# First transfers of an attention and two-MLP kernel cut smaller, weight splits moved to other turns

## What is computed

```python
scores = np.where(mask, scale * q @ k.T, -1e9)          # mask: 0 <= i - j < 64
attn = exp(scores - max); attn = attn / (sum(attn) + 1e-9)
x = attn @ v                                             # as 1152 x 512
h = x @ w_in
x = (np.maximum(h, 0) + np.log1p(np.exp(-np.abs(h)))) @ w_out
p = domain_probs / (domain_probs.sum(-1) + 1e-9)
out = sum(p[:, e:e+1] * (np.maximum(x @ w1[e], 0) @ w2[e]) for e in range(4))
```

## Time and profile before

| | us |
|---|---|
| median of 3 runs (lowest, highest) | 632.37 (631.67, 632.61) |
| the profiled execution | 631.56 |
| its span, first to last instruction | 629.8 |
| TensorE busy | 621.8 (99%) |
| VectorE busy | 388.0 (62%) |
| ScalarE busy | 276.7 (44%) |
| GpSimd busy | 88.9 (14%) |

### The profile page before, as it was taken

How to read it: one execution, slowest core, us unless ns; L and a number is a source line. 1 busy time by engine, 2 the same in 40 slices (tenths; PEclk the granted TensorE clock), 3 DMA queues, 4 the chain that set the end, 5 groups by cost and what they waited for, 6 DMA issues and landing times.

```text
span 629.8 us, 10144 instructions
## 1 busy us (share of the span) xinstructions
PE 621.8 (99%) x3892; PEld 579.0 (92%) x3892; DVE 388.0 (62%) x840; ACT 276.7 (44%) x635; POOL 88.9 (14%) x92
## 2 busy tenths in 40 slices
PE   8999999999999999999999999999999999999998
PEld 7789999999999999998998988988988988988987
DVE  5896674577646588887277277276276376376342
ACT  6986765566445455552342332332332432432410
POOL 2653333323333332000000000000000000000000
PEclk9999999999999999999999999999999999999999
DMA  8814130123100010022102103003003003000012
GB/s 330 348 68 193 69 135 1 35 100 138 64 2 0 1 35 34 1 68 101 35 0 101 34 1 104 31 1 110 25 1 122 12 2 131 4 0 1 1 51 100
DMA packets 10704, 40.78 MB, mean 65 GB/s; under 512 B 1312, under 2 KB 1568, under 8 KB 9376
## 3 DMA queue, kind: packets, MB, share of 16 engines
q1 hardware_dynamic: 10656, 40.13, 17.7%
HBM read 37.77 MB, written 2.36 MB: 64 GB/s over the span
## 4 chain that ended last, share of the span: by engine, by line
PE 94%; ACT 1%; DVE 1%; DMA 1%; issue 1%; SPq 0%; POOL 0%; DVEq 0%; ACTq 0%
PE banks L1123 31%; PE banks L1099 28%; PE banks L1068 16%; PE banks L1048 15%; PE banks L1035 1%; DMA unit_in<-in_units 1%; PE banks L1009 1%; PE banks L1022 1%; ACT prob L498 1%; PE banks L1115 0%; DVE sp_l L734 0%; DVE prob L684 0%; ACT hid_hi L539 0%; ACT probT L507 0%; ACT sp_l L534 0%
## 5 line engine op out<-in xcount | busy, mean ns | idle before, releaser
L1123 PE MATMUL banks<-wb_hi,ehid_hi 128*128 128x512 f32 x284 | 110.5, 389 | 0.0
L1123 PE MATMUL banks<-wb_lo,ehid_hi 128*128 128x512 f32 x284 | 110.5, 389 | 0.0
L1123 PE MATMUL banks<-wb_hi,ehid_lo 128*128 128x512 f32 x284 | 110.5, 389 | 0.0
L431 POOL TENSOR_TENSOR sp_c<-sp_e,sp_c 128x384 f32<-128x384 f32 x48 | 63.6, 1324 | 135.3 <-DVE sp_c L720 135.3
L862 DVE SCALAR_TENSOR_TENSOR part<-banks,gate,part 128x512 f32<-128x512 f32 x62 | 46.6, 751 | 54.0 <-PE banks L1123 54.0
L1099 PE MATMUL banks<-T_lo,aop_hi 128*128 128x288 f32 x256 | 75.6, 295 | 0.0
L1099 PE MATMUL banks<-T_hi,aop_lo 128*128 128x288 f32 x256 | 75.6, 295 | 0.0
L1099 PE MATMUL banks<-T_hi,aop_hi 128*128 128x288 f32 x256 | 75.3, 294 | 0.0
L1068 PE MATMUL banks<-hid_hi,wb_hi 128*128 128x384 f32 x192 | 65.8, 342 | 0.8 <-DVE wb_lo L672 0.7
L1048 PE MATMUL banks<-xy_hi,wa_hi 128*128 128x384 f32 x192 | 66.3, 345 | 0.0
L1068 PE MATMUL banks<-hid_hi,wb_lo 128*128 128x384 f32 x192 | 64.3, 335 | 0.0
(11 more groups left out here) (106 smaller groups left out, 1247.5 us busy)
## 6 DMA issues: line engine op xcount, KB each, us to landing
unit_in<-in_units SPq DMA_DIRECT2D x8, 1024.0 KB, 6.3
raw_a<-in_w SPq DMA_DIRECT2D x16, 512.0 KB, 3.3
raw_b<-in_w SPq DMA_DIRECT2D x16, 512.0 KB, 3.3
raw_a<-in_w_in SPq DMA_DIRECT2D x8, 512.0 KB, 6.0
raw_b<-in_w_out SPq DMA_DIRECT2D x8, 512.0 KB, 4.2
part<-in_units SPq DMA_DIRECT2D x2, 1024.0 KB, 12.1
out_dram<-part SPq DMA_DIRECT2D x8, 256.0 KB, 2.0
unit_in<-in_units SPq DMA_DIRECT2D x2, 384.0 KB, 7.7
```

The source lines that it names most:

```text
L431: pool.tensor_tensor(sp_c[:, s, :], sp_e[:, s, :], sp_c[:, s, :], ALU.subtract).then_inc(lost_done, 1)
L1123: m = pe.matmul(TOKEN_BANKS[T], ehid[x][:, i, P * T:P * T + P], wb[a][:, f, :], start=(i == 0 and j == 0), stop=(i == 3 and j == 2))
```

## The change

1. In memory, a unit's keys (256 columns) now stand in front of its queries (384). Unit 0's inputs come in two pieces: keys and the first window's queries (192 KB), then the other queries (128 KB). Units 1, 2 and 3 each have a transfer of 320 KB. Groups 2 and 3 come in two pieces each, 640 KB and 384 KB, with the values later.
2. Unit 0's three windows go into three banks, and TensorE counts `first_scores` behind windows 0 and 1, so VectorE masks each window by itself.
3. The high copies of `wa` move from the turns 4, 5, 7, 8, 9 to 5, 6, 8, 9 and a last one behind turn 9, and GpSimd's epsilons and low halves move with them.
4. GpSimd waits in step 0 for unit 10's normalisation, and does block 4's second half in step 1. Block 5 is split by ScalarE in step 1 and by GpSimd in step 2, no longer by ScalarE and VectorE in step 3.
5. VectorE does `activation(0, 0)` in step 1, behind masked_scores(11).

```diff
-SPLIT_GROUPS = 2
+SPLIT_GROUPS = 4
+SINGLE = 4
+FIRST_QK = UNIT + WIN + P
...
+        def score_block(u, w):
+            bank = (score_bank(0), ps[1], ps[2])[w] if u == 0 else score_bank(u)
+            return bank[:, P * w:P * w + P]
...
-        FIRST_SPLIT = {4: 0, 5: 1, 7: 2, 8: 3, 9: 4}
+        FIRST_SPLIT = {5: 0, 6: 1, 8: 2, 9: 3}
-        LATE_SPLIT = {3: 5, 4: 6, 5: 7}
+        LATE_SPLIT = {4: 6, 5: 7}
...
-            sp.dma_start(slots[0][:, 0:UNIT_QK], units[0][:, 0:UNIT_QK]).then_inc(first_unit_landed, 16)
-            sp.dma_start(slots[0][:, UNIT_QK:2 * UNIT_QK], units[0][:, UNIT_QK:2 * UNIT_QK]).then_inc(scores_landed[0], 16)
-            first_queries_keys(1)
+            sp.dma_start(slots[0][:, 0:FIRST_QK], units[0][:, 0:FIRST_QK]).then_inc(first_window_landed, 16)
+            sp.dma_start(slots[0][:, FIRST_QK:UNIT_QK],
+                         units[0][:, FIRST_QK:UNIT_QK]).then_inc(unit_scores_landed[0], 16)
+            for u in range(1, SINGLE):
+                unit_queries_keys(u)
             first_values(0)
-            attention_inputs(2)
+            first_queries_keys(2)
             first_values(1)
-            attention_inputs(3)
+            first_queries_keys(3)
+            first_values(2)
             up_weights(0, up_in(0), (0,))
             attention_inputs(4)
+            first_values(3)
             up_weights(0, up_in(0), (1,))
...
-            for u in (2, 3, 4):
+            for u in (2, 3, 4, 5):
                 add_eps(u)
-            for i, unit in enumerate((4, 5, 6, 7)):
-                add_eps(unit + 1)
-                if unit in FIRST_SPLIT:
+            for i, unit in enumerate((5, 6, 7, 8)):
+                if unit + 1 in EPS_AHEAD:
+                    add_eps(unit + 1)
+                if i < 2:
                     pool.wait_ge(wa_hi, FIRST_SPLIT[unit] + 1)
                 else:
                     pool.wait_ge(norm_done, unit + 1)
                 up_low_half(i // 2, i % 2)
...
+            for i in range(4, 8):
+                pool.wait_ge(norm_done, SCORED)
+                if i % 2 == 0:
+                    pool.wait_ge(wa_hi, i // 2 + 1)
                 up_low_half(i // 2, i % 2)
             for k in range(STEPS):
                 lost(k // FT, k % FT)
                 if k == 0:
+                    pool.wait_ge(norm_done, SCORED + 1)
                     pool.wait_ge(wb_hi, 1)
                     down_low_half(0)
                     down_low_half(1)
-                    pool.wait_ge(wa_hi, len(FIRST_SPLIT))
-                    up_low_half(len(FIRST_SPLIT) - 1, 0)
-                    up_low_half(len(FIRST_SPLIT) - 1, 1)
+                    pool.wait_ge(wa_hi, 5)
+                    up_low_half(4, 0)
                 elif k < N_UNITS - SCORED:
                     normalise(k + SCORED)
+                if k == 1:
+                    up_low_half(4, 1)
+                elif k == 2:
+                    pool.wait_ge(wa_hi, 6)
+                    up_low_half(5, 0)
+                    up_low_half(5, 1)
...
+                if k == 1:
+                    act.wait_ge(wa_hi, 5)
+                    split_up(0, 5)
...
+                    if u == 0 and w < 2:
+                        dve.wait_ge(first_scores, w + 1)
+                    elif u == 0:
+                        dve.wait_ge(score_done, 1)
...
+            up_high(4)
...
+                if k == 1:
+                    activation(0, 0)
...
+                    if u == 0 and w == 1:
+                        pe.wait_ge(unit_scores_landed[0], 16)
+                    if u == 0 and w < 2:
+                        m.then_inc(first_scores, 1)
```

More of the change, by code:

```diff
@@ L189, in two_stage_mlp_after_window_attention @@
         qk_slots = [i[:, 0:2 * UNIT_QK].rearrange("p (t n) -> p t n", t=2) for i in slots]
-        q_slots = [i[:, :, 0:3 * P].rearrange("p t (w c) -> p t w c", w=3) for i in qk_slots]
-        k_slots = [i[:, :, 3 * P:UNIT_QK] for i in qk_slots]
+        q_slots = [i[:, :, UNIT + WIN:UNIT_QK].rearrange("p t (w c) -> p t w c", w=3) for i in qk_slots]
+        k_slots = [i[:, :, 0:UNIT + WIN] for i in qk_slots]
         v_slots = [i[:, Q_COLS + K_COLS:SLOT].rearrange("p (w c) -> p w c", w=3) for i in slots]
@@ L242, in two_stage_mlp_after_window_attention @@
         unit_landed = [sem(f"unit_landed{i}") for i in range(SLOTS + EARLY)]
-        scores_landed = [sem(f"scores_landed{g}") for g in range(SPLIT_GROUPS)]
-        first_unit_landed = sem("first_unit_landed")
+        scores_landed = {g: sem(f"scores_landed{g}") for g in (2, 3)}
+        first_window_landed = sem("first_window_landed")
+        unit_scores_landed = [sem(f"unit_scores_landed{u}") for u in range(SINGLE)]
         gate_in = sem("gate_in")
@@ L250, in two_stage_mlp_after_window_attention @@
         negmax_done = sem("negmax_done")
+        first_scores = sem("first_scores")
         first_maxima = sem("first_maxima")
@@ L319, in _, with unit_queries_keys @@
             QK = Q_COLS + K_COLS
+            def unit_queries_keys(u):
+                cols = slice(UNIT_QK * (u % 2), UNIT_QK * (u % 2) + UNIT_QK)
+                sp.dma_start(slots[u // 2][:, cols], units[u // 2][:, cols]).then_inc(unit_scores_landed[u], 16)
             def first_queries_keys(g):
@@ L458, in _ @@
                 up_low_half(i // 2, i % 2)
-            for i, unit in zip(range(len(FIRST_SPLIT) - 1, 2 * len(FIRST_SPLIT) - 2), (8, 9, 9, 9)):
-                pool.wait_ge(norm_done, unit + 1)
-                if i == 4:
-                    pool.wait_ge(wa_hi, 3)
-                elif i == 6:
-                    pool.wait_ge(wa_hi, 4)
+            for i in range(4, 8):
+                pool.wait_ge(norm_done, SCORED)
+                if i % 2 == 0:
+                    pool.wait_ge(wa_hi, i // 2 + 1)
                 up_low_half(i // 2, i % 2)
@@ L675, in masked_scores @@
             def masked_scores(u):
-                dve.wait_ge(score_done, u + 1)
+                if u > 0:
+                    dve.wait_ge(score_done, u + 1)
                 if u >= 3:
@@ L683, in masked_scores @@
                     m = 0 if first and w == 0 else 1
-                    e = dve.tensor_tensor_reduce(prob[:, u % 3, w, :], score_bank(u)[:, P * w:P * w + P],
+                    if u == 0 and w < 2:
+                        dve.wait_ge(first_scores, w + 1)
+                    elif u == 0:
+                        dve.wait_ge(score_done, 1)
+                    e = dve.tensor_tensor_reduce(prob[:, u % 3, w, :], score_block(u, w),
                                                  mask[:, m, :], -SCALE, BIG, ALU.add, ALU.min,
@@ L911, in _ @@
                         x_low(k + WEIGHED)
-                activation(n, f)
+                if k > 0:
+                    activation(n, f)
                 if n >= 1 and f == LAG - 1:
@@ L1000, in scores @@
                 if u == 0:
-                    pe.wait_ge(first_unit_landed, 16)
+                    pe.wait_ge(first_window_landed, 16)
+                elif u < SINGLE:
+                    pe.wait_ge(unit_scores_landed[u], 16)
                 elif u < 2 * SPLIT_GROUPS:
@@ L1008, in scores @@
                 for w in range(3):
-                    m = pe.matmul(score_bank(u)[:, P * w:P * w + P], q_slots[s][:, u % 2, w, :],
+                    if u == 0 and w == 1:
+                        pe.wait_ge(unit_scores_landed[0], 16)
+                    m = pe.matmul(score_block(u, w), q_slots[s][:, u % 2, w, :],
                                   k_slots[s][:, u % 2, WIN * w:WIN * w + P], start=True, stop=True)
+                    if u == 0 and w < 2:
+                        m.then_inc(first_scores, 1)
                 m.then_inc(score_done, 1)
@@ L1214 @@
                 v, 1 - h, 0)[3 * u:3 * u + 3, :, P * hp0:P * hp0 + 2 * P].transpose(1, 0, 2)
-        qk[:, :, :3 * P] = qh.reshape(P, 2, 3 * P)
-        qk[:, :, 3 * P:] = np.roll(k, WIN - UNIT * u, 2)[hp0:hp0 + 2, :, :UNIT + WIN].transpose(1, 0, 2)
+        qk[:, :, UNIT + WIN:] = qh.reshape(P, 2, 3 * P)
+        qk[:, :, :UNIT + WIN] = np.roll(k, WIN - UNIT * u, 2)[hp0:hp0 + 2, :, :UNIT + WIN].transpose(1, 0, 2)
         at[:, :Q_COLS + K_COLS] = qk.reshape(P, 2 * UNIT_QK)
```

## The result

The changed kernel took 632.61 us (median of 22 runs, 632.21 to 635.0); the kernel before, run beside it, 632.10 (22 runs, 631.42 to 632.99).

What follows compares the result with a forecast made beforehand. TensorE, busy 621.8 of 629.8 us, bounds the kernel; only gains ahead of its group at 45.65, waiting on VectorE, count. 0.60 - 0.15 = 0.45 us earlier gives 631.1 profiled, plus 0.81 for the median: 631.9; range 630.7 to 633.2.

Steps and rivals of the forecast that it cites:

- Unit 0: Start of kernel: VectorE's first mask starts behind the first window, 0.45 us sooner; lead at unit 0's maxima 0.43.
- Units 2 and 4: First transfers: smaller pieces land unit 2 near 6.3 and unit 4 at 10.1; lead 0.54, then 0.9 us.
- Units 4 to 7: Exponentials on ScalarE: unit 4 at 12.5, 1.75 us a unit, unit 7 at 17.75; lead 1.2 us.
- the second rival: Early lead under about 0.7 at unit 7, low halves come late; end 0.65 to 1.3 us later; chance 0.15.
- the wait on `wa_lo`: Sign: TensorE waits about 1 us on `wa_lo` ahead of `start_up(0, 0)` at 20.2.
- the late cast: Sign: third `raw_a` issued near 24.2, VectorE's cast at about 27.6, where 26.8 was before.
- unit 4's scores at 10.1: Sign: TensorE starts unit 4's scores near 10.1 us, a lead of 0.9.
- unit 7's exponentials at 17.7: Sign: ScalarE's exponentials of unit 7 come near 17.7 us, a lead of 1.2.
- Where the lead goes: GpSimd's low halves behind later units: scores(9) unchanged, third `raw_a` issued 0.9 us later; lead becomes a lag of 0.9.
- (a): Step 0: GpSimd waits for unit 10's normalisation, VectorE's epsilon and normalisation shorten; gain 0.84 us, lag left 0.05.
- (b): Step 1: `activation(0, 0)` behind mask 11 brings the mask earlier, but `split_up(0, 5)` delays unit 11's exponential; gain 0.
- (c): Block 5's low half moves from VectorE's step 3 to GpSimd's step 2: 0.60 us gained, 0.15 cost.

Runs made afterwards that it cites:

- e17: Kernel before with only unit 0's scores put in three banks and counted window by window; ratio to before 1.0001.
- e4: Changed kernel with both GpSimd low halves of a block together, the second ahead of the next unit's epsilon; 631.83 us, ratio to before 1.0002.
- e10: e4 with block 5 split in step 3 by ScalarE and VectorE as before the change; 631.92 us, ratio to before 0.9997.
- e2: Changed kernel's order on all engines (casts, low halves, late steps, block 5), but the kernel before's transfers; 633.08 us, ratio to before 1.0024.
- e7: Kernel before with block 1's second low half on GpSimd right behind its first, ahead of unit 8's epsilon; ratio to before 1.0.
- e1: Kernel before plus GpSimd's wait for unit 10's normalisation, `activation(0, 0)` behind mask 11, and block 5's low half off VectorE's step 3; ratio 1.0001.
- e6: e1 with block 5 split by ScalarE and VectorE in step 3 as in the kernel before; 631.26 us, ratio to before 0.999.
- e11: e3 plus GpSimd's wait for unit 10's normalisation, block 4's second half in step 1 and `activation(0, 0)` behind mask 11; 631.12 us, ratio 0.9987.
- e18: e6 plus unit 0's scores counted by windows, every transfer as in the kernel before; 631.12 us, ratio to before 0.9987.
- e9: Changed kernel with block 5 split in step 3 by ScalarE and VectorE as before the change; 632.74 us, ratio to before 1.0013.
- e12: e3 with group 1's queries and keys in one transfer of 640 KB; ratio to before 1.0006.
- e14: Kernel before with unit 0's queries and keys in two pieces, plus keys-first layout and scores by windows; ratio to before 1.0006.
- e15: e11 with unit 0's queries and keys in one whole transfer; 630.84 us, ratio to before 0.9987.
- e13: e3 with unit 0's queries and keys in one transfer of 320 KB; ratio to before 0.9989.
- e3: Kernel before with only the change's smaller transfers and unit 0 in two pieces with scores by windows; ratio to before 0.9998.
- e5: e3 with SyncE held back from issuing more until unit 2's inputs have landed; ratio to before 1.0018.
- e8: e3 and e7 together: the change's transfers plus block 1's second low half right behind its first; ratio to before 0.9997.

## Why the prediction was wrong

**Unit 0: right.** 0.43 us were forecast for the first maxima; the mask came 0.47 sooner, and e17 gets 0.42 without any piece (5.41): the windows do it, not the transfer. Single profiles spread here as well: 5.49 to 6.26 in six kernels without the windows, 4.92 to 5.63 in the fourteen with them.

**Units 2 and 4: wrong, and the cause of the rest.** This is the step that failed: a lead of 0.9 us at unit 4 was forecast, and there is none (its exponentials start at 13.45, 13.41 before). "It lands near 6.3" was the rate of the kernel before taken over to a different list of transfers. Unit 2 landed at 7.72, and TensorE got it at 7.77. That alone took the lead: TensorE came to unit 4's scores only at 10.94 and waited 0.17 more, where 10.1 was forecast. The prediction had noted "any landing up to 6.9 gives the same" and had the slow stretch in hand (0.30 MB a microsecond) as an argument for the rival; it didn't carry it into its sum. The rule that it had weighed, in the Trainium skill's "DMA: Bandwidth & Descriptors", section Bandwidth, that small copies be batched, was put aside with rows from behind 11 us, where 384 to 1024 KB pieces run at the full rate in the changed kernel too (421 GB/s from 8.5 to 17 us, 426 before). It was the wrong stretch to test it in: from 4.5 to 6.5 us the same pieces cost a third of the rate (211 GB/s for 313). This fits the page as far as its direction goes; why two such edits don't add up, no run here shows.

**Units 4 to 7: the pace right, the start wrong.** 1.75 us a unit were forecast, and from 13.45 to 18.65 it is 1.73, against 1.85 before (13.41 to 18.96). So the casts in later turns bring the 0.3 that is left. Lead at unit 7: 1.2 forecast, 0.3 measured. With 0.3 put in place of 1.2, the prediction's own chain gives what happened: `wa_lo` 1 at 21.0 (measured 21.03), the third `raw_a` issued 0.9 later than the 24.25 forecast, at 25.15 (25.28). This is the second rival, "the later halves cost", whose point was a lead under 0.7 and whose end, 0.65 to 1.3 later, holds the 1.1 of the profile. It had 0.15. Of the signs that the prediction gave, the wait on `wa_lo` and the late cast came, but they come with the lead and without it; those that tell, unit 4's scores at 10.1 and unit 7's exponentials at 17.7, did not.

**Where the lead goes: right in kind.** The order by which GpSimd's half stands behind a later unit's epsilon and normalisation works as written, and e4, e10 and e2 show it by undoing it or keeping it alone. "TensorE starts scores(9) when it did before" rested on the lead: they start at 21.73, 0.91 later (20.82). In the changed kernel mask 10 does wait for the cast (29.21), the path that the prediction followed. A second path lies close behind, which it didn't look at: `start_up(0, 0)` and `start_up(1, 0)` wait for `wa_lo`, and the scores of unit 10 come 1.54 later (27.84 for 26.30), which with e7's 0.87 lets the mask start at 28.71. So a sooner transfer alone could give back 0.5 us here and 0.3 in the kernel before (e7), not the whole wait for `raw_a`.

**(a): right.** Unit 10's maxima end 1.71 us late and its normalisation 0.87 late: 0.84 gained, as forecast. What was missed is that the meeting moves on: `rounded` 0.35 to 0.89 and epsilon 11 0.17 to 0.84 in the changed kernel, 0.90 and 0.86 in e1, 0.89 and 0.93 in e6. In the changed kernel the activations of step 1 are 1.21 late where the normalisation was 0.87: 0.3 us of the 0.84 went back. The Trainium skill's "SBUF — State Buffer", section Who interferes with whom, says more than the prediction took from it: VectorE's `tensor_scalar` too can take the port pair that VectorE shares with GpSimd, and whichever of the two issues second is blocked for the whole instruction of the first. The trace agrees: the epsilon, a `tensor_scalar`, loses 0.67 us beside a `lost` of 0.99 that began 0.17 before it. So a pair that is moved apart has to be followed to what it meets next.

**(b): right, near 0.** Unit 11's first exponential comes at 33.72, 0.70 late under a normalisation 0.87 late, and the epsilon behind it 0.68 late (35.00 for 34.32). The pause of 0.33 that VectorE had there is used up by the longer `rounded`. With the low halves in their old places (e6, e11, e18) part 4 as a whole is worth 0.1%.

**(c): size off.** 0.60 gained, 0.15 cost by the forecast. Measured: the activation of step 3 ends 0.49 later than that of step 2 would have it (1.70 against 1.21 late), by `hidden_low` 1.09 (0.55 before) and an epsilon of 0.51, both under GpSimd's two low halves and the `lost` pushed back by them. Net 0.1: the cost is the upper bound of 0 to 0.5 and not the 0.15 taken. e6 against e1 and e9 against the changed kernel show no gain by part 5 either.

**Sum** for the profile: 1.71 - 0.84 + 0.34 - 0.11 = 1.10 us, what the group at 46.75 and the span show, where -0.45 was forecast: 1.71 late at unit 10's maxima less the 0.84 of (a), plus what went back, less the net of (c). The two misses are the lag at unit 10 (1.71 where 0.9 was forecast), which is the missing lead, and the net of (c) with the 0.34 (0.45 and 0 forecast); the prediction's sum also left out its own lag of 0.05. The median of many runs moved less than this pair of profiles, 0.8 us by the ratio. That the time lies inside the range is due to the range, not to the account.

## What to carry to other kernels

When transfers are cut up, take the rate from the stretch in which they will run, the first microseconds above all, and not from the steady stream. A step written to stand behind a later unit spends its lead first and may cost more than the lead ever was. Work out the lead that it needs before counting what is gained ahead of it, and follow every engine that waits for it, not only the first. Moving one of two engines that disturb each other moves the meeting, so the gain stands only when the next pair has been looked at.

## What the runs showed of the hardware

- Between 4.5 and 6.5 us the stream of the first transfers ran at 301 to 339 GB/s with 320, 320 and 640 KB in front (eight profiles), at 252 with the first of these cut in two (e12, e14), at 177 and 206 with the 640 KB and later ones cut (e15, e13), and at 211 to 244 with both (changed kernel, e3, e4, e5, e8 to e11), while the DMA engines' share fell only from 0.96 before to 0.85 in the changed kernel. From 8.5 to 17 us all have 403 to 426 (398 where SyncE was held).
- In the same 2 us each packet took 59 to 68 ns longer than in the steady stream, at 5120 bytes (255 ns in the kernel before, 196 in the steady stream of e13) as at 2560 (164 in the changed kernel and 170 in e13, where it is 102 from 6.5 to 7.5 us); over all profiles it is 37 to 93 ns.
- SyncE's issues took 0.33 to 0.46 us each in the quiet and 0.53 to 0.79 between 4 and 7.5 us (changed kernel); held back, they changed the stream by some 0.2 us (e5).
- GpSimd's presence costs VectorE's small instructions most in proportion: the epsilon goes from 0.17 us to 0.51, 0.84 (changed kernel) or 0.93 (e6), `rounded` from 0.35 to 0.90 (e1), the cast from 0.42 to 0.80, `hidden_low` from 0.55 to 1.09.
- In 6 of the 20 profiles group 4 landed at 19.3 to 20.4 us and in the others at 17.6 to 18.6, with the same transfers ahead of it (19.43 in e2, where TensorE waits 1.2 us for it, and 18.21 in e1). The six executions took 631.99 to 632.78 us and 636.03 (e5), the fourteen others 630.73 to 632.64, all but three of them at most 631.6. What decides in which execution this occurs stays open.
- In e5's execution, behind two waits of TensorE of 0.97 and 1.17 us within 3.3 us, the granted clock was 1.2 GHz for 6.8 us (2.4 before and after), and the time was 3.4 us above the median of its runs.
